# Sparse attention and two feed-forward layers on one core: an unrolled program with another order of slots

## The chip, the cores and the metric

The kernel runs on one core of a Trainium2 chip. Its time is the device time of that core in microseconds (us). The kernel before took 1284.62 us, the median of three runs (1283.78 to 1285.82). Every instruction duration below comes from one profiled execution of it.

## The reference

Four batches of eight heads with 576 tokens each and head dimension 64. Each row of scores keeps its 32 largest values; the rest get weight zero.

```
scores = (q @ k.T) / 8
kth    = partition(scores, -32)[..., -32]          # the 32nd largest of each row
scores = where(scores >= kth, scores, -1e9)
attn   = exp(scores - max) / (sum(exp(scores - max)) + 1e-9)
x  = (attn @ v) laid out as 2304 tokens x 512
h  = x @ w_in ;  g = h - tanh(h) ;  y = g @ w_out       # first feed-forward, 512 -> 2048 -> 512
h2 = y @ w_in2 ; g2 = elu(h2)    ;  out = g2 @ w_out2   # second feed-forward
```

Everything is in float32. The large products are made of three float32r products each (high by high, low by high, high by low), so every tensor that enters one is split into a high and a low part.

## The kernel before

The program has two phases. In the first, attention and the first feed-forward layer run side by side, in slots written out by hand; in the second, the second feed-forward layer runs alone (`h2`, `y2`, line 683 and line 728) over four groups of 512 tokens and one of 256.

A **unit** of attention is one tile of 128 queries of one head, against 576 keys; there are 144, one to a slot. The 64 queries that are left over in each head are gathered into tail units. Nine slots make a round, and each engine walks through its own list of every slot:

- TensorE (`round_`): turn the weights of unit u-3 with five transposes (`turn_weights`, lines 579 and 580), scores of unit u+1 (lines 563 and 564), some pieces of the first layer (`h_part` line 611, `y_part` line 626, transposes of g, line 653, and of x, line 647), and last weights by values of unit u-3 (`attend`, line 598).
- VectorE: four MAX8 and three MATCH_REPLACE8 find the 32 largest scores (lines 964, 973, 979, 984, 993, 1005). A reciprocal of the weight sum, which comes out of the product with an added column of ones, is line 989. It also makes h - tanh(h) for two of four blocks (line 998).
- ScalarE: exp of unit u-2 (line 821), copies out of PSUM (scores line 782, the rest through `high`, line 755), tanh (line 833), scaling of the attention's result by the reciprocal (line 865).
- GpSimd: the mask, scores >= 32nd (line 1104), exp times mask (line 1110), and low parts (lines 1076, 1092, 1122, 1131).

An engine runs its list strictly in its order; semaphores hold it where it needs another's result. The exp and the mask of a unit are made one slot before TensorE turns its weights. Steady slots are in loops (`Fori`); a tile of 128 tokens goes through the first layer in nine slots, with 512-wide products.

Of the kernel before, what the change touches and what calls it, by code (L numbers as in the profile page):

```python
# [6 lines left out]
F32R = mybir.dt.float32r  # L28
ALU = mybir.AluOpType
# [4 lines left out]
LOWEST = -3.0e38  # L34
EPS = 1e-9
# [5 lines left out]
def after(eng, sem, count):  # L41

    if not (isinstance(count, int) and count <= 0):
        eng.wait_ge(sem, count)


def apart(eng, passed):


    eng.sem_inc(passed)  # L50


class Round:

    def __init__(self, rho, batch, pair, rounds, units=True, refill=False, fresh=False, left=True, new=True, old=True):
        self.rho, self.batch, self.pair, self.refill, self.fresh = rho, batch, pair, refill, fresh
        self.pair_before = (pair + 3) % 4
        self.units, self.left, self.new, self.old = units, left, new, old
        self.more = units and not (isinstance(rho, int) and rho == rounds - 1)

    def has(self, u):

        if u < 0:
            return self.left
        return self.units if u < 9 else self.more


def each_round(eng, step, batches, tails):

    per = 4
    n = batches * per
    step(Round(0, 0, 0, n, left=False, new=False, old=False))  # L80
    step(Round(1, 0, 1, n, old=False))
    step(Round(2, 0, 2, n))
    step(Round(3, 0, 3, n, refill=True))
    with eng.Fori(1, batches - 1) as b:
        step(Round(b * per, b, 0, n, fresh=True))
        with eng.Fori(1, per - 1) as r:
            step(Round(b * per + r, b, r, n))
        step(Round(b * per + per - 1, b, per - 1, n, refill=True))
    step(Round(n - per, batches - 1, 0, n, fresh=True))
    with eng.Fori(1, per - 1) as r:  # L90
        step(Round(r + (n - per), batches - 1, r, n))
    step(Round(n - 1, batches - 1, per - 1, n))
    step(Round(n, batches, 0, n, units=False))
    for i in range(tails):
        step(Round(n + 1 + i, batches, 0, n, units=False, left=False))
    step(Round(n + 1 + tails, batches, 0, n, units=False, left=False, new=False))


def build(nc, qT, kT, v, w1_in, w1_out, w2_in, w2_out, out):
# [21 lines left out]
    with ctx:  # L121
# [131 lines left out]

        W2_SLOTS = {1: (0, 1, 2, 3)}
        OUT_AHEAD = 2

# [929 lines left out]
```

## Time and profile before

| | |
|---|---|
| median of 3 runs | 1284.62 us |
| span of the profiled execution | 1281.9 us |
| TensorE busy | 1203.8 us (94%) |
| VectorE busy | 896.5 us (70%) |
| ScalarE busy | 702.2 us (55%) |
| GpSimd busy | 790.3 us (62%) |
| first product of the second layer starts | 872.38 us |

The span leaves out about 3 us around the first and the last instruction. The busy share of TensorE is an upper figure: its matmuls overlap, and their modelled durations are longer than the distance from one start to the next. So distances between starts are what prices a product. Until about 780 us VectorE is full as well; after 872 us only TensorE is.

### The profile page before, as it was taken

Reading aid. Unit: us, or ns where it says so; the run is one execution under the profiler, and the core shown is the slowest. Engines: PE = TensorE matmul, PEld = TensorE weight load, DVE = VectorE, ACT = ScalarE, POOL = GpSimd, SP = SyncE. Lnnn points to the kernel's source line nnn. Section 1 sums busy time; section 2 is a strip of 40 time slices with the busy share of each in tenths; the row PEclk is TensorE's granted clock in tenths of the full one; section 3 lists DMA queues with packets and bytes.
Section 4 is the critical chain, followed back from the end, with each engine's and each line's share of the span. In section 5 each row is a group of like instructions: output and inputs, shape, how many; then the busy total and the mean of one; then the engine's idle time right before and its main releaser. Section 6 shows DMA issues by size and latency. Waiting matters only on the chain.

```text
span 1281.9 us, 23141 instructions
## 1 busy us (share of the span) xinstructions
PE 1203.8 (94%) x6784; PEld 1039.2 (81%) x6784; DVE 896.5 (70%) x1870; ACT 702.2 (55%) x1534; POOL 790.3 (62%) x579
## 2 busy tenths in 40 slices
PE   3678999999998999999999999999999999999997
PEld 2667887888887888888888888788888888888887
DVE  7999999999999999999999995015532222222221
ACT  5667777766776766777766765345432222222221
POOL 4898888888987888988888986332222222222221
PEclk9679999999999999999999999999999999999999
DMA  6410022000022100022000000504001001010000
GB/s 201 168 56 13 20 62 75 30 21 22 23 68 64 32 21 21 25 66 68 28 26 13 21 11 12 188 12 170 1 1 66 1 1 65 0 50 1 1 33 17
DMA packets 46420, 56.81 MB, mean 44 GB/s; under 512 B 13296, under 2 KB 28656, under 8 KB 45808
## 3 DMA queue, kind: packets, MB, share of 16 engines
q1 hardware_dynamic: 46320, 55.59, 13.7%
q8 instruction: 48, 0.79, 0.2%
q14 instruction: 52, 0.43, 0.1%
HBM read 45.61 MB, written 9.96 MB: 43 GB/s over the span
## 4 chain that ended last, share of the span: by engine, by line
PE 71%; issue 12%; DVE 6%; ACT 5%; POOL 4%; DVEq 0%; DMA 0%; ACTq 0%; POOLq 0%; SPq 0%
PE ps L683 15%; PE ps L728 15%; PE ps L611 11%; PE ps L626 10%; PE ps L598 9%; PE ps L579 4%; PE ps L563 2%; PE ps L564 2%; PE ps L653 2%; DVE best L973 1%; POOL keep L1104 1%; DVE work L1005 1%; DVE best L964 1%; PE ps L580 1%; ACT kT_hi_over_lo L755 1%
## 5 line engine op out<-in xcount | busy, mean ns | idle before, releaser
L1104 POOL TENSOR_SCALAR keep<-scores,best 128x576 f32<-128x576 f32 x144 | 253.6, 1761 | 58.3 <-DVE best L964 55.9
L1148 POOL TENSOR_TENSOR elu_lo<-elu_h,elu_hi 128x512 fp32r<-128x512 f32 x72 | 92.9, 1290 | 305.7 <-ACT elu_hi L755 305.7
L598 PEld LDWEIGHTS ps<-v_and_one,weights_T 128*128 128x128 f32 (+1 forms) x1440 | 183.5, 198 | 56.0 <-issue 49.3
L598 PE MATMUL ps<-v_and_one,weights_T 128*128 128x129 f32 (+2 forms) x1440 | 196.1, 285 | 34.9 <-ACT x L865 33.0
L1110 POOL TENSOR_TENSOR kept_weights<-work,keep 128x576 f32<-128x576 f32 x144 | 205.9, 1430 | 26.8 <-POOL keep L1104 17.8
L964 DVE MAX8 best<-work 128x8 f32<-128x576 f32 x288 | 213.8, 742 | 0.2
L1043 DVE TENSOR_SCALAR exp_h<-exp_h 128x512 f32<-128x512 f32 x72 | 30.7, 427 | 239.9 <-ACT exp_h L907 239.9
L755 ACT ACTIVATE weights_T<-ps 128x512 f32<-128x512 f32 (+1 forms) x288 | 115.1, 433 | 118.6 <-PE ps L580 105.1
L907 ACT ACTIVATE exp_h<-ps 128x512 f32<-128x512 f32 x72 | 43.1, 598 | 194.3 <-PE ps L683 194.3
L821 ACT ACTIVATE work<-scores,exp_bias 128x576 f32<-128x576 f32 x144 | 111.6, 775 | 24.4 <-DVE best L964 24.0
L563 PE MATMUL ps<-kT_hi_over_lo,qT_hi 128*128 128x288 f32 (+1 forms) x320 | 106.1, 347 | 20.1 <-DVE kT_hi_over_lo L937 15.5
L1122 POOL TENSOR_TENSOR gT_lo<-gT_raw,gT_hi 128x512 fp32r<-128x512 f32 x72 | 92.5, 1285 | 45.9 <-ACT gT_hi L755 45.1
L626 PE MATMUL ps<-w_out_hi,gT_hi 128*128 128x512 f32 x288 | 115.7, 402 | 2.8 <-POOL gT_lo L1122 2.5
L683 PE MATMUL ps<-yT_hi,w_in_hi 128*128 (+2 forms) x320 | 117.8, 368 | 0.0
L683 PE MATMUL ps<-yT_lo,w_in_hi 128*128 (+2 forms) x320 | 117.8, 368 | 0.0
L683 PE MATMUL ps<-yT_hi,w_in_lo 128*128 (+2 forms) x320 | 117.7, 368 | 0.0
L611 PE MATMUL ps<-w_in_hi,xT_hi 128*128 128x512 f32 x288 | 115.4, 401 | 0.0
L728 PE MATMUL ps<-w_out_hi,elu_hi 128*128 128x512 f32 x288 | 113.6, 395 | 1.1 <-POOL elu_lo L1148 1.1
L973 DVE MAX8 best<-scores 128x8 f32<-128x576 f32 x144 | 108.4, 753 | 8.0 <-ACT scores L782 4.7
L611 PE MATMUL ps<-w_in_hi,xT_lo 128*128 128x512 f32 x288 | 112.9, 392 | 0.0
L611 PE MATMUL ps<-w_in_lo,xT_hi 128*128 128x512 f32 x288 | 112.8, 392 | 0.0
L626 PE MATMUL ps<-w_out_lo,gT_hi 128*128 128x512 f32 x288 | 112.5, 391 | 0.0
(83 smaller groups left out, 2880.7 us busy)
## 6 DMA issues: line engine op xcount, KB each, us to landing
kT_raw<-kT SPq DMA_DIRECT2D x64, 144.0 KB, 2.8
w_in_raw<-w_in SPq DMA_DIRECT2D x8, 1024.0 KB, 7.5
w_out_raw<-w_out SPq DMA_DIRECT2D x8, 1024.0 KB, 5.5
qT_raw<-qT SPq DMA_DIRECT2D x64, 96.0 KB, 2.5
ffn_rows<-act SPq DMA_DIRECT2D x18, 256.0 KB, 2.1
v_and_one<-v SPq DMA_DIRECT2D x16, 256.0 KB, 2.7
rows<-ffn_rows SPq DMA_DIRECT2D x4, 1024.0 KB, 6.5
out<-out_rows SPq DMA_DIRECT2D x16, 256.0 KB, 2.4
```

The costliest lines, as they stand in the source:

```text
L563: pe.matmul(ps[:, half, 0:HALF], q_hi[:, slot, :], rhs, start=(n == 0), stop=False)
L598: mm = pe.matmul(ps[:, B_OUT, 0:2 * D + 1], pt[0:k, c, :], rhs, start=(c == 0), stop=(c == FULL))
L611: mm = pe.matmul(ps[:, B_H + fb % 2, :], l[:, kc, :], r[:, kc, ws], start=(kc == 0 and n == 0), stop=(kc == KC - 1 and n == 2))
L626: mm = pe.matmul(ps[:, B_Y, :], l[:, fb % 2, c, :], r[:, fb * CPB + c, :], start=(fb == 0 and c == 0 and n == 0), stop=(fb == FB - 1 and c ...
L683: mm = pe.matmul(ps[:, B_H + f % 2, j * n * P:(j + 1) * n * P], l[:, kc, cs], r(kc), start=(kc == 0 and i == 0), stop=(kc == KC - 1 and i ...
L728: mm = pe.matmul(ps[:, t, :], l[:, f % 2, ts], r[:, c, :], start=(c == 0 and i == 0), stop=(c == FC - 1 and i == 2))
L755: return nc.scalar.activation(out_, in_, ACT.Copy)
L821: nc.scalar.activation(wk[:, i, :], sc[:, i, :], ACT.Exp, bias=nbias[:, i:i + 1], scale=SCALE).then_inc(exped, 1)
L964: nc.vector.max(best[:, u % 3, n * EIGHT:(n + 1) * EIGHT], wk[:, u % 3, :]).then_inc(chain_old, 1)
L973: nc.vector.max(best[:, i, 0:EIGHT], sc[:, i, :]).then_inc(chain_new, 1)
L1104: nc.gpsimd.tensor_scalar(keep[:, :], sc[:, i, :], best[:, i, TOP - 1:TOP], None, ALU.is_ge).then_inc(kept, 1)
L1110: nc.gpsimd.tensor_tensor(kept_w[:, :], wk[:, i, :], keep[:, :], ALU.mult).then_inc(masked, 1)
```

## The change

The whole program is written anew, without loops. There are again 144 attention slots (128 head tiles, 16 tail units, four of these after the first tile of each batch), numbered from 0.

- **Mask.** The comparison and the product with the mask are gone. GpSimd makes two small differences per unit (`biases`: minus the 32nd score, and the 32nd score minus the maximum); ScalarE runs a Prelu over the scores with the first as bias and a slope of 1e30 below zero (`cut_scores`), then exp in place, which also gives the sum of the weights (`exp_scores`, `accum_out`). GpSimd adds 1e-9 (`sum_eps`), VectorE inverts (`invert`), GpSimd multiplies the weights by the inverse (`norm`).
- **Order of a slot on TensorE:** scores of the next unit, attend of a finished pair, one chunk of h, one chunk of y, and last the turn of the weights.
- **Values.** attend runs for a pair of heads at once, with 64 columns of values as the stationary operand and the turned weights streaming, into upper and lower halves of one bank. Its result is x already transposed, so the transposes of x are gone.
- **First layer.** h comes out transposed, for two tiles at a time (256 columns streaming); the transposes of g are gone. One chunk of h and one of y per slot, in slots 24 to 168: 144 chunks.
- **Elsewhere.** The low parts of the first weights are all made by GpSimd, two in each of slots 5 to 20; the low parts of the keys of later batches by GpSimd too (24). The copy of scores applies the scale. The second layer's own steps stay the same; half of its weights' splits are placed elsewhere.

The core of the difference, TensorE's list of a slot and the new steps:

```diff
-                for u in range(U):
-                    if rd.has(u - 3):
-                        turn_weights(rd, u - 3)
-                    if rd.has(u + 1) and rd.units:
-                        scores(rd, u + 1)
-                    for step, fb, first, end, which in steps(rd, u):
...
-                    if rd.has(u - 3):
-                        attend(rd, u - 3)
+            for s in range(-1, LAST + 1):
+                done, old, new = unit(s - 3), unit(s - 2), unit(s + 1)
+                if new:
+                    scores(new)
+                if done and done.ends_pair:
+                    attend(done)
+                if s in h_in:
+                    h_step(h_in[s])
+                if s in y_in:
+                    y_step(y_in[s])
+                if old:
+                    turn_weights(old)
```

```diff
-                        nc.gpsimd.tensor_scalar(keep[:, :], sc[:, i, :], best[:, i, TOP - 1:TOP], None, ALU.is_ge
-                                                ).then_inc(kept, 1)
...
-                        nc.gpsimd.tensor_tensor(kept_w[:, :], wk[:, i, :], keep[:, :], ALU.mult).then_inc(masked, 1)
+            def cut_scores(u):
+                sc_e.wait_ge(biased, u.t + 1)
+                nc.scalar.activation(sc[:, u.t % 4, :], sc[:, u.t % 4, :], ACT.Prelu, bias=bias[:, u.t % 2, 0:1],
+                                     scale=1.0, alpha=STEEP).then_inc(cut, 1)
+            def exp_scores(u):
+                sc_e.wait_ge(cut, u.t + 1)
+                after(sc_e, summed, u.t - 1)
+                nc.scalar.activation(sc[:, u.t % 4, :], sc[:, u.t % 4, :], ACT.Exp, bias=bias[:, u.t % 2, 1:2],
+                                     scale=1.0, accum_out=sums[:, u.t % 2:u.t % 2 + 1]).then_inc(exped, 1)
+            def norm(u):
+                po.wait_ge(inverted, u.t + 1)
+                w = sc[:, u.t % 4, :]
+                nc.gpsimd.tensor_scalar(w, w, rinv[:, u.t % 2:u.t % 2 + 1], 1.0, ALU.mult, ALU.mult).then_inc(normed, 1)
+            def turn_weights(u):
+                pe.wait_ge(normed, u.t + 1)
```

```diff
+            def attend(u):
...
+                        mm = pe.matmul(ps[half * D:(half + 1) * D, B_OUT, cols], values[:, half * D:(half + 1) * D],
+                                       weights, start=(c == 0), stop=(c == FULL))
+            def h_step(i):
...
+                for kc in range(KC):
+                    for n, (l, r) in enumerate(((win_hi, xt_hi), (win_lo, xt_hi), (win_hi, xt_lo))):
+                        mm = pe.matmul(ps[:, B_H + i % 2, 0:N], l[:, kc, fs], r[:, kc, ring:ring + N],
+                                       start=(kc == 0 and n == 0), stop=(kc == KC - 1 and n == 2))
```

ScalarE's list, one steady slot of the kernel before (loops' register rows are among them). `work` is the exp, `weights_T` the turned weights of the unit before it, `gT` the first layer's g:

```order
L815 ACTIVATE exp_bias<-best 128x1 [waits chain_new]
L819 ISA
L821 ACTIVATE work<-scores,exp_bias 128x576 [waits biased,chain_old]
L755 ACTIVATE weights_T<-ps 128x512 [waits attended,turned]
L839 REGISTER_ALU
L755 ACTIVATE weights_T<-ps 64x128 [waits scored]
L755 ACTIVATE gT_raw<-ps 128x512 [waits y_done,g_turned]
L755 ACTIVATE gT_hi<-ps 128x512
L865 ACTIVATE x<-ps,sum_inverse 128x64 [waits inverted]
```

And of the changed kernel, from the cut of a unit (L607) to the cut of the next:

```order
L607 ACTIVATE scores<-scores,exp_bias 128x576 [waits biased]
L580 ACTIVATE gT_hi<-gT_raw 128x256 [waits g_done]
L613 ACTIVATE scores,weight_sum<-scores,exp_bias 128x576 [waits summed,cut]
L602 ACTIVATE scores<-ps 128x576 [waits turned,scored]
L580 ACTIVATE gT_raw<-ps 128x256 [waits y_done,h_done]
L647 ACTIVATE tanh_h<-ps 128x256
L580 ACTIVATE weights_T<-ps 128x512 [waits attended,turned]
L580 ACTIVATE weights_T<-ps 64x128
L607 ACTIVATE scores<-scores,exp_bias 128x576 [waits biased]
```

The copy of turned weights stood behind the exp of a younger unit; now it is the last step of the slot in which the same unit was cut and exponentiated, and the next unit's cut stands behind it.

GpSimd's list in the same place, one slot of the kernel before (the mask of a unit, then its weights):

```order
L1104 TENSOR_SCALAR keep<-scores,best 128x576 [waits chain_old,masked]
L1107 REGISTER_ALU
L1110 TENSOR_TENSOR kept_weights<-work,keep 128x576 [waits kept,turned,exped]
L1119 REGISTER_ALU
L1122 TENSOR_TENSOR gT_lo<-gT_raw,gT_hi 128x512 [waits split_high]
```

And of the changed kernel, a slot in which queries are split too:

```order
L907 TENSOR_TENSOR gT_lo<-gT_raw,gT_hi 128x256 [waits g_high]
L893 TENSOR_SCALAR weight_sum_eps<-weight_sum 128x1 [waits inverted,exped]
L861 TENSOR_TENSOR qT_lo<-qT_raw,qT_hi 128x256 [waits q_high]
L898 TENSOR_SCALAR scores<-scores,sum_inverse 128x576 [waits inverted]
L902 TENSOR_TENSOR gT_raw<-gT_raw,tanh_h 128x256 [waits tanh_done]
L886 TENSOR_TENSOR exp_bias<-best 128x2 [waits exped,chain_late]
```

Where one full-width pass took the threshold from VectorE and the other the exp from ScalarE, the one full-width pass (L898) now waits for VectorE's reciprocal, which waits for L893.

TensorE in a slot that ends a pair, changed kernel (`v_rows` and `v_rest` are the values):

```order
L436 MATMUL ps<-kT_hi_over_lo,qT_hi 128x288 [waits copied,k_split,q_split]
L437 MATMUL ps<-kT_hi_over_lo,qT_lo 128x288
L436 MATMUL ps<-kT_hi_over_lo,qT_hi 128x288
L437 MATMUL ps<-kT_hi_over_lo,qT_lo 128x288
L464 MATMUL ps<-weights_T,v_rows 64x128 [waits x_out,turned_copied,v_in2]
L464 MATMUL ps<-weights_T,v_rows 64x128 x7
L464 MATMUL ps<-weights_T,v_rest 64x128 x2
L483 MATMUL ps<-xT_hi,w_in_hi 128x256 [waits turned_copied,tanh_done]
```

The turn of the weights has moved from the head of the slot to its end, and attend, ten products every second slot in place of five in each, from the end to behind the scores.

## Rows read from the trace of the kernel before

**Rows 1.** The page: span, and busy time by engine.

```profile
span 1281.9 us, 23141 instructions
PE 1203.8 (94%) x6784; PEld 1039.2 (81%) x6784; DVE 896.5 (70%) x1870; ACT 702.2 (55%) x1534; POOL 790.3 (62%) x579
```

**Rows 2.** Stretches: width, busy us and instructions by engine, TensorE's granted clock, DMA, GB/s.

```profile
40.00:80.00 40.00, 28.11 (x134) 25.25 (x134) 39.34 (x82) 26.35 (x61) 37.70 (x27) 0.63 0.37 131
...
480.00:520.00 40.00, 39.36 (x258) 35.21 (x257) 40.00 (x91) 28.20 (x68) 35.73 (x26) 1.00 0.06 18
```

**Rows 3.** The chain that ended last, in order of time: start, us, what.

```profile
486.32 0.44 PE ps L579 x4
...
487.40 2.74 PE ps L611 x12
490.14 0.44 PE ps L653 x4
490.57 1.12 PE ps L598 x10
```

**Rows 4.** The same chain, where the second layer begins.

```profile
872.38 2.77 PE ps L683 x12
```

**Rows 5.** VectorE in order of time: start, busy us, operation; first unit, then one steady unit.

```profile
10.27 0.76 DVE L973 MAX8 best<-scores 128x8 f32<-128x576 f32 x1 [0.30 <-ACT scores L782]
...
500.48 0.75 DVE L973 MAX8 best<-scores 128x8 f32<-128x576 f32 x1
...
505.37 0.74 DVE L973 MAX8 best<-scores 128x8 f32<-128x576 f32 x1
```

**Rows 6.** ScalarE by line and shape: count, busy us, mean ns.

```profile
L821 ACT ACTIVATE work<-scores,exp_bias 128x576 f32<-128x576 f32 x144 | 111.6, 775 | 24.4 <-DVE best L964 24.0
L755 ACT ACTIVATE weights_T<-ps 128x512 f32<-128x512 f32 x144 | 85.9, 597 | 106.2 <-PE ps L580 105.1
L833 ACT ACTIVATE act<-ps 128x512 f32<-128x512 f32 x72 | 42.7, 592 | 4.5 <-PE ps L611 4.4
L755 ACT ACTIVATE weights_T<-ps 64x128 f32<-64x128 f32 x144 | 38.7, 269 | 12.4 <-PE ps L564 12.4
L755 ACT ACTIVATE qT_hi<-qT_raw 128x256 fp32r<-128x256 f32 x16 | 6.7, 419 | 0.0
```

**Rows 7.** GpSimd and VectorE by line and shape.

```profile
L1104 POOL TENSOR_SCALAR keep<-scores,best 128x576 f32<-128x576 f32 x144 | 253.6, 1761 | 58.3 <-DVE best L964 55.9 <-POOL kept_weights L1110 1.4 <-POOL kT_hi_over_lo L1092 0.9
L1076 POOL TENSOR_TENSOR qT_lo<-qT_raw,qT_hi 128x256 fp32r<-128x256 f32 x16 | 12.2, 763 | 0.0
L1133 POOL MEMSET qT_hi<- 128x256 f32 x1 | 0.3, 311 | 0.3 <-POOLq L1183 0.3
L989 DVE RECIPROCAL sum_inverse<-ps 128x1 f32<-128x1 f32 x144 | 22.5, 156 | 10.3 <-PE ps L598 10.3
```

**Rows 8.** GpSimd, two low parts of weights.

```profile
37.38 2.84 POOL L1131 TENSOR_TENSOR w_in_lo<-w_in_raw,w_in_hi 128x512 fp32r<-128x512 f32 x2 [3.36 <-ACT w_in_hi L755]
```

**Rows 9.** Hand-overs from engine to engine, in order of time.

```profile
499.10 0.74 DVE L964 MAX8 best<-work 128x8 f32<-128x576 f32 x1
...
500.07 1.72 POOL L1104 TENSOR_SCALAR keep<-scores,best 128x576 f32<-128x576 f32 x1 [0.79 <-DVE best L964]
...
501.46 0.27 PE L580 MATMUL ps<-ident,kept_weights 128*64 128x128 f32 x1
501.85 0.75 ACT L755 ACTIVATE weights_T<-ps 128x512 f32<-128x512 f32 x2 [1.20 <-PE ps L580]
...
1226.59 0.63 ACT L755 ACTIVATE elu_hi<-elu_h 128x512 fp32r<-128x512 f32 x1 [1.22 <-DVE elu_h L1048]
1227.30 1.29 POOL L1148 TENSOR_TENSOR elu_lo<-elu_h,elu_hi 128x512 fp32r<-128x512 f32 x1 [4.15 <-ACT elu_hi L755]
```

**Rows 10.** TensorE, 256-column products of the last group; the 1st and the 13th.

```profile
1227.30 0.28 PE L683 MATMUL ps<-yT_hi,w_in_hi 128*128 128x256 f32 x1
...
1228.73 0.28 PE L683 MATMUL ps<-yT_hi,w_in_hi 128*128 128x256 f32 x1
```

More of the change, by code:

```diff
@@ L34 @@
 LOWEST = -3.0e38
+STEEP = 1.0e30
 EPS = 1e-9
@@ L41, in after, with __init__, plan @@
 def after(eng, sem, count):
-    if not (isinstance(count, int) and count <= 0):
+    if count > 0:
         eng.wait_ge(sem, count)
[L47 to L96, printed above, removed]
+class Unit:
+    def __init__(self, t, batch, tile, head=None, pair=None):
+        self.t, self.batch, self.tile, self.head, self.pair = t, batch, tile, head, pair
+        self.tail = head is None
+        self.ends_pair = self.tail or head % 2 == 1
+def plan(batches, per, heads):
+    units = []
+    for b in range(batches):
+        for r in range(per):
+            for h in range(heads):
+                units.append(Unit(len(units), b, b * per + r, head=h, pair=h // 2))
+            if r == 0:
+                for p in range(heads // 2):
+                    units.append(Unit(len(units), b, None, pair=p))
+    return units
 def build(nc, qT, kT, v, w1_in, w1_out, w2_in, w2_out, out):
@@ new lines, in build @@
+    last_unit_of = {u.tile: u.t for u in units if not u.tail}
+    for u in units:
+        if u.tail:
+            last_unit_of[R + u.batch // 2] = u.t
+    tiles = sorted(range(TILES), key=last_unit_of.get)
+    seq_of = {tile: j for j, tile in enumerate(tiles)}
+    RING = 4
+    GN = 2
+    GROUPS = TILES // GN
+    N = GN * P
+    CHUNKS = GROUPS * FC
+    READY = 5
+    h_slot = []
+    for g in range(GROUPS):
+        first = max(last_unit_of[tiles[g * GN + GN - 1]] + READY, h_slot[-1] + 1 if h_slot else 0)
+        h_slot += range(first, first + FC)
@@ L720, in y2 @@
                     after(pe, res_dve, g * (CPB // 2))
-                if isinstance(g, int) and g == 0:
+                if g == 0:
                     pe.wait_ge(w2o_split, f + 1)
@@ new lines, in copy_x @@
+            def copy_x(u):
+                e = event_of[u.t]
+                sc_e.wait_ge(attended, e + 1)
+                if u.tail:
+                    half = u.batch % 2
+                    if u.pair == 0 and half == 0 and u.batch > 0:
+                        sc_e.wait_ge(x_split, seq_of[R + u.batch // 2 - 1] + 1)
+                    to = tail_raw[:, u.pair, half * D:(half + 1) * D]
+                    high(to, ps[:, B_OUT, 0:D]).then_inc(x_out, 1)
+                else:
+                    if u.pair == 0 and u.tile > 0:
+                        sc_e.wait_ge(x_split, seq_of[u.tile - 1] + 1)
+                    high(tile_raw[:, u.pair, :], ps[:, B_OUT, 0:P]).then_inc(x_out, 1)
```

1151 lines of the change are left out of this document (501 added, 650 removed).

## The prediction

> **What bounds the kernel now.** I read the page's busy times first, then the table of stretches, then the chain of waits in order of time, and last the engines' own timelines for the distance between starts. TensorE is busy for 94% of the span and VectorE for 70% [rows 1]. In a stretch in the middle of the first phase both are full: VectorE 40.00 of 40.00 us, TensorE 39.36, at the full clock [rows 2]. The chain there is nothing but TensorE: from a turn to the end of the next attend 5.37 us (486.32 to 491.69), made of 1.08 for the turn and the scores (486.32 to 487.40), 2.74 for twelve 512-column products, 0.44 for turning g and 1.12 for ten passes of attend [rows 3]. One unit costs VectorE 4.89 us (500.48 to 505.37) where no block of g falls to it [rows 5]. So a slot is worth 5.0 to 5.4 us, held by TensorE with VectorE close behind; ScalarE and GpSimd have room, and no unit's exp, mask and turn fall into one slot. The first unit starts at 10.27 [rows 5], the second layer at 872.38 [rows 4]; its remaining 409.5 us stay as they are.
>
> **TensorE's and VectorE's work in the changed kernel.** Thirteen starts of 256-column products lie 1.43 us apart over twelve [rows 10], so a chunk of h costs 1.43. A chunk of y is six products at 2.74/12 = 0.228, 1.37. With turn and scores 1.08 and attend at the old price, 1.12 a unit, a slot holds 5.0 us of TensorE: as much as before, since the saved transposes (0.44, two or three times in nine slots) are paid for by 256-column products, which cost 0.119 for half of what costs 0.228. VectorE keeps seven passes and a reciprocal, 4.89, and loses the blocks of g. If these two set the pace, the kernel gains. I don't think they do.
>
> **The wait that the order adds.** In the changed kernel ScalarE's list of a slot begins with the cut of a unit and ends with the copy of that same unit's turned weights, and the next unit's cut stands behind that copy. Between them lies everything: cut, exp, sum, reciprocal, norm, turn, copy. That is a closed loop of one slot, and its length is a sum of rows:
> cut 0.68 (0.775, Prelu priced as exp, less the 0.10 by which neighbours overlap in the pair of copies of [rows 9]: 0.75 for 0.597 + 0.269); high part of g 0.32 (0.419 less 0.10); exp 0.775 [rows 6]; its sum 0.15, which no row shows: I take half of the smallest copy, 0.269, with 0 and 0.27 as ends; hand-over to GpSimd 0.08 (1226.59 + 0.63 to 1227.30 [rows 9]); the addition on 128 x 1 an estimated 0.20 (the 128x256 row, 0.763, is the nearest above); hand-over 0.08; reciprocal 0.156 [rows 7]; VectorE to GpSimd 0.23 (499.84 to 500.07 [rows 9]); norm n; hand-over 0.08; turn 0.71 (0.44 for four [rows 3] and the fifth's 0.27); to ScalarE 0.12 (501.73 to 501.85); copies 0.67. Sum: 4.25 + n.
> For n, a one-tensor pass of 576 elements on GpSimd, the rows give 1.761 for the comparison, also one tensor and a pointer, as the upper end, and for the lower a memset scaled from 256 to 576 elements, 0.70 [rows 7]. A product needs no comparison; I take 1.3. The loop is then 5.55 us, over both engines' work.
> That functions cost the same on ScalarE is in [rows 6]: tanh on 512 elements 592 ns, copy 597. So Prelu's price is hardly in doubt.
> The page GPSIMD Engine Reference of the Trainium skill (section Engine selection) says that one-input passes on GpSimd are "roughly line-rate". The trace disagrees for the comparison: 1.761 for 576 elements is 3.1 ns an element [rows 7], and a two-input subtraction of 512, 1.29 us, is 2.5 [rows 9]. With a line-rate norm of about 0.6 us, an estimate from that page, the time below would be near 1365.
>
> **Two kinds of slots.** Odd slots: the low part of the queries, 0.763, stands in GpSimd's list between the sum and the norm, where only 0.47 (0.08 + 0.156 + 0.23) is free, so they cost 0.30 more, 5.85. Even slots end a pair: TensorE, after its turn, waits for the copy (0.12 + 0.77 + 0.08), then attend, h, y and turn follow in a row: 0.97 + 1.43 + 1.37 + 0.71 = 4.48 plus attend. Twenty passes at 1.12/10 make 2.24, if halves of the array don't work at once, 1.12 if they do. No row shows two column halves side by side. I take 1.6, between the ends: 6.08. The mean is 5.96 us a slot.
> TensorEngine Tiling (Array Packing) in the Trainium skill (section Key Properties) says that different tiles of the array run independently; by that rule attend costs 1.12 and the sum is that of the first rival below. No row here shows it either way.
>
> **The sum.** Slots 0 to 4 and 21 to 23, without g: 5.23 each, 42. Slots 5 to 20: GpSimd makes two low parts of weights, 2.84 [rows 8], between norm and the next biases, so its own loop is 2.84 + 0.25 (biases, estimate) + 0.08 + cut 0.83 + exp 0.93 + 0.08 + 0.20 + 0.08 + 0.16 + 0.23 + 1.3 = 6.98, times 16 = 112. With the start at 10.3, slot 24 begins at 164. Slots 24 to 145: 122 x 5.96 = 727. To these come the low parts of 24 keys, priced as one of a weight, 1.42 each [rows 8], and again between sum and norm: 15 fall on odd slots in full, 9 on even ones for about 0.4, 25 us; and 16 low parts of x at 1.29 (the 512-wide row of [rows 9]), all on odd slots, 21. Attention ends at 937. Then 22 slots hold h and y alone: work 2.80, and the way h, tanh, difference, high part, low part, y about 3.0, which with two buffers makes 2.9 a slot, 64; last y 1.4; then 409.5. Together 1412 on the profiled execution's clock; the median lies 2.7 over the span [rows 1], so 1415 us.
> Edits priced at nothing: the longer list of ScalarE, 3 us of it inside its wait for the turn, which is 3.4 long; splits of the second weights, two passes on ScalarE and two on VectorE a slot in the last 12 slots, where VectorE has nothing else to do; queries' and values' loads on SP, waited for two slots or more after issue; the loops' register work, saved, on engines that have time. If ScalarE's cover is gone, in slots with keys (1.2 more), the cost is some tenths on 24 slots, under 10 us.
>
> **Rivals.**
> *Halves side by side and a cheap norm* (0.17): even slots 5.60, odd ones 5.25 at n = 0.7, and about the same fixed parts less 12: near 1340 with no price for the sum, 1389 where n stays 1.3. For it: nothing in the trace forbids either. Against it: each needs the lower end.
> *The loop doesn't bind, VectorE does* (0.08, the side on which the kernel is faster): if ScalarE's and GpSimd's steps overlap more than their rows do, a slot costs VectorE's 4.89 and 146 of them end at 10 + 714 + 20 for the slots with weights = 744; with 64 + 1.4 + 409.5 + 2.7 that is 1222 us. The place is ScalarE's copy of turned weights, and it decides from a mean of 5.27 us over slots 24 to 145, extras included: (1284.6 - 2.7 - 409.5 - 65.4 - 164)/122. Against it: 4.25 + n gives 4.95 even at n = 0.70, and queries, keys and x come on top of that in the same place.
> *No overlap and a dear norm* (0.15): attend 2.24, n = 1.761: even 6.72, odd 6.31, 122 x 6.52 = 795, start 11 more: 1490 us.
> *The clock falls* (0.04): TensorE would be idle for 15 to 20% of each slot. In 40 to 80 us, with 28.11 of 40 busy, the granted clock was 0.63 of full speed [rows 2], which is the 1.2 GHz level for much of it. At that level the slot's 5.0 us become 10: every ten slots add 40 us, so over 1500. Against it, such stretches would have to last.
>
> **How the numbers follow.** Forecast 0.56: the loop binds, with prices between the ends. It gives 1415. Range 1340 to 1490, from the low ends of norm and attend to their high ends, which leaves out the fast rival and the clock. What a measurement can tell from no change is 0.2%, about 2.6 us. Slower: 0.91, that is forecast, first, third and fourth rival, less 0.01 for a mean slot that lands just on 5.27. Faster 0.08, same 0.01.
>
> **What would show it.** Right: in the profile after, VectorE idles before each reciprocal, about 0.7 to 1.1 us, waiting for GpSimd; ScalarE idles before the copy of turned weights, released by TensorE's turn; TensorE idles before the turn in odd slots, released by GpSimd's norm; starts of MAX8 on scores lie 5.8 to 6.1 apart. The chain walks cut, exp, norm, turn, copy. Slots 5 to 20 are near 7 us. The norm's mean and the distance of attend's passes decide the size. Wrong: VectorE full between 170 and 900 us, or a chain that is all TensorE.

## The result and the profile after

| | before | changed |
|---|---|---|
| median, us | 1284.2 (1282.85 to 1285.82, 4 runs) | 1471.07 (1469.05 to 1472.4, 4 runs) |
| ratio to before | | 1.1458, 95% interval 1.1442 to 1.1474 |
| profiled execution: span, us | 1281.9 | 1467.2 |
| mean granted clock of TensorE | 0.980 | 0.934 |

The kernel became 14.6% slower. The forecast was 1415 us, its range 1340 to 1490.

The page of the changed kernel: busy time by engine, then three groups of the page (busy us, mean ns | idle before, releaser).

```profile
PE 1214.2 (83%) x7448; PEld 1001.5 (68%) x7448; DVE 846.8 (58%) x1796; ACT 767.9 (52%) x1792; POOL 624.1 (43%) x968
...
L580 ACT ACTIVATE weights_T<-ps 128x512 f32<-128x512 f32 (+1 forms) x288 | 108.2, 427 | 220.1 <-PE ps L448 220.1
...
L447 PE MATMUL ps<-ident,scores 128*128 128x128 f32 x576 | 101.5, 304 | 121.5 <-POOL scores L898 121.0
...
L792 DVE RECIPROCAL sum_inverse<-weight_sum_eps 128x1 f32<-128x1 f32 x144 | 23.5, 163 | 202.9 <-POOL weight_sum_eps L893 202.9
...
L898 POOL TENSOR_SCALAR scores<-scores,sum_inverse 128x576 f32<-128x576 f32 x144 | 108.4, 753 | 25.1 <-DVE sum_inverse L792 23.9
```

Against [rows 1]: TensorE's work is nearly the same (1214.2 us for 1203.8), VectorE's, ScalarE's and GpSimd's together is 150 us less, and the span is 185 us longer: 177 of it ahead of the second layer, whose first product starts at 1049.40 and not 872.38 [rows 4], and 8 in it. In the attention slots no engine is full any more. The three waits that the prediction named are all there: ScalarE before the copy of turned weights (220.1 us), TensorE before the turn (121.5), VectorE before the reciprocal (202.9).

The stretches that answer to [rows 2], one in the slots with weights' splits and one in the middle:

```profile
120.00:160.00 40.00, 20.48 (x135) 16.65 (x134) 32.05 (x72) 28.27 (x62) 25.30 (x38) 0.59 0.04 11
...
480.00:520.00 40.00, 31.12 (x216) 25.39 (x216) 28.34 (x62) 29.61 (x71) 21.62 (x36) 0.91 0.18 52
```

VectorE, 40.00 of 40 before in the second of them, is at 28.34.

One odd slot in the changed kernel, from ScalarE's cut to the next. These are lines of the trace in order of time, each engine's own (start, busy us, operation, idle before it and who ended it). ScalarE:

```profile
437.48 0.75 ACT L580 ACTIVATE weights_T<-ps 128x512 f32<-128x512 f32 x2 [1.28 <-PE ps L448]
438.13 0.77 ACT L607 ACTIVATE scores<-scores,exp_bias 128x576 f32<-128x576 f32 x1
438.80 0.41 ACT L580 ACTIVATE gT_hi<-gT_raw 128x256 fp32r<-128x256 f32 x1
439.11 0.77 ACT L613 ACTIVATE scores<-scores,exp_bias 128x576 f32<-128x576 f32 x1
439.77 0.20 ACT L613 ACTIVATION_READ_ACCUMULATOR scores<-scores,exp_bias 128x1 f32 x1
...
442.73 0.75 ACT L580 ACTIVATE weights_T<-ps 128x512 f32<-128x512 f32 x2 [1.69 <-PE ps L448]
443.38 0.77 ACT L607 ACTIVATE scores<-scores,exp_bias 128x576 f32<-128x576 f32 x1
```

GpSimd, with the low part of the queries (L861) between sum and norm:

```profile
440.11 0.21 POOL L893 TENSOR_SCALAR weight_sum_eps<-weight_sum 128x1 f32<-128x1 f32 x1
440.40 0.74 POOL L861 TENSOR_TENSOR qT_lo<-qT_raw,qT_hi 128x256 fp32r<-128x256 f32 x1
441.12 0.75 POOL L898 TENSOR_SCALAR scores<-scores,sum_inverse 128x576 f32<-128x576 f32 x1
```

TensorE, the even slot before and this odd one's turn:

```profile
432.42 1.09 PE L464 MATMUL ps<-weights_T,v_rows 128*64 128x128 f32 x16 [0.36 <-issue]
433.44 0.44 PE L464 MATMUL ps<-weights_T,v_rest 64*64 64x128 f32 x4
433.81 0.39 PE L483 MATMUL ps<-xT_hi,w_in_hi 128*128 128x256 f32 x1
...
435.35 0.40 PE L497 MATMUL ps<-w_out_hi,gT_hi 128*128 128x512 f32 x1
...
436.74 0.60 PE L447 MATMUL ps<-ident,scores 128*128 128x128 f32 x4
...
441.93 0.66 PE L447 MATMUL ps<-ident,scores 128*128 128x128 f32 x4 [0.19 <-POOL scores L898]
```

Odd slot: copy done 438.13, cut, high part, exp from 439.11, accumulator read to 439.97, sum at 440.11, queries' low part, norm at 441.12, turn at 441.93, copy at 442.73, next cut at 443.38: 5.25 us, all of it one strand through ScalarE, GpSimd and TensorE. Even slot: copy 431.57 (not shown), attend 432.42, h 433.81, y 435.35, turn 436.74, copy 437.48: 5.91, and from the copy on it is TensorE's own work. Between the cuts of slots 24 and 145 lie 121 distances. 77 of them are plain: mostly 5.2 and 5.9 us in turn, 4.8 to 6.1 in all. The other 44, all above 6.2, are treated below. One unit took 4.89 before [rows 5].

### The profile page after: what moved, and what is told of

Read it like the earlier page. It is cut to its first block, busy times and chain, and to the rows that moved or that the text cites. A ratio compares the mean times of both kernels' runs of the same rounds, so it can differ in the third digit from the quotient of the medians.

```text
span 1467.2 us, 21851 instructions
## 1 busy us (share of the span) xinstructions
PE 1214.2 (83%) x7448; PEld 1001.5 (68%) x7448; DVE 846.8 (58%) x1796; ACT 767.9 (52%) x1792; POOL 624.1 (43%) x968
## 4 chain that ended last, share of the span: by engine, by line
PE 34%; POOL 29%; issue 26%; ACT 3%; DVE 3%; SPq 2%; DMA 1%; POOLq 0%; ACTq 0%
PE ps L544 13%; PE ps L527 13%; POOL gT_lo L907 6%; POOL scores L898 6%; POOL gT_raw L902 5%; POOL qT_lo L861 3%; PE ps L497 2%; POOL kT_hi_over_lo L868 2%; PE ps L483 2%; POOL weight_sum_eps L893 2%; PE ps L464 2%; POOL exp_bias L886 1%; POOL xT_lo L880 1%; DVE best L776 1%; DVE work L785 1%
## 5 line engine op out<-in xcount | busy, mean ns | idle before, releaser
L580 ACT ACTIVATE weights_T<-ps 128x512 f32<-128x512 f32 (+1 forms) x288 | 108.2, 427 | 220.1 <-PE ps L448 220.1
L785 DVE MATCH_REPLACE8 work<-best,work 128x576 f32<-128x576 f32 x288 | 213.9, 743 | 0.0
L447 PE MATMUL ps<-ident,scores 128*128 128x128 f32 x576 | 101.5, 304 | 121.5 <-POOL scores L898 121.0
L483 PE MATMUL ps<-xT_hi,w_in_hi 128*128 128x256 f32 x576 | 177.2, 308 | 22.4 <-ACT weights_T L580 22.4
L483 PE MATMUL ps<-xT_hi,w_in_lo 128*128 128x256 f32 x576 | 165.3, 287 | 0.0
L483 PE MATMUL ps<-xT_lo,w_in_hi 128*128 128x256 f32 x576 | 164.9, 286 | 0.0
L436 PE MATMUL ps<-kT_hi_over_lo,qT_hi 128*128 128x288 f32 x320 | 115.2, 373 | 42.1 <-POOL qT_lo L861 27.5
L483 PEld LDWEIGHTS ps<-xT_hi,w_in_hi 128*128 128x128 f32 x576 | 112.1, 195 | 45.0 <-issue 37.3
L792 DVE RECIPROCAL sum_inverse<-weight_sum_eps 128x1 f32<-128x1 f32 x144 | 23.5, 163 | 202.9 <-POOL weight_sum_eps L893 202.9
L607 ACT ACTIVATE scores<-scores,exp_bias 128x576 f32<-128x576 f32 x144 | 110.8, 770 | 27.5 <-POOL exp_bias L886 27.5
L527 PE MATMUL ps<-yT_hi,w_in_hi 128*128 128x512 f32 (+1 forms) x320 | 119.8, 374 | 0.0
L527 PE MATMUL ps<-yT_lo,w_in_hi 128*128 128x512 f32 (+1 forms) x320 | 119.3, 373 | 0.0
L898 POOL TENSOR_SCALAR scores<-scores,sum_inverse 128x576 f32<-128x576 f32 x144 | 108.4, 753 | 25.1 <-DVE sum_inverse L792 23.9
L527 PE MATMUL ps<-yT_hi,w_in_lo 128*128 128x512 f32 (+1 forms) x320 | 119.1, 372 | 0.0
```

The costliest lines, as they stand in the source:

```text
L436: pe.matmul(ps[:, half, 0:HALF], q_hi[:, n % QRING, lhs], rhs, start=(i == 0), stop=False)
L447: pe.transpose(ps[:, B_TURN, c * P:(c + 1) * P], w[:, c * P:(c + 1) * P], ident[:, :])
L483: mm = pe.matmul(ps[:, B_H + i % 2, 0:N], l[:, kc, fs], r[:, kc, ring:ring + N], start=(kc == 0 and n == 0), stop=(kc == KC - 1 and n == 2))
L527: mm = pe.matmul(ps[:, B_H + f % 2, j * n * P:(j + 1) * n * P], l[:, kc, cs], r[:, buf, kc, 0:n * P], start=(kc == 0 and i == 0), stop=(kc ...
L607: nc.scalar.activation(sc[:, u.t % 4, :], sc[:, u.t % 4, :], ACT.Prelu, bias=bias[:, u.t % 2, 0:1], scale=1.0, alpha=STEEP).then_inc(cut, 1)
L785: nc.vector.match_replace(wk[:, u.t % 2, :], best[:, u.t % 3, 1 + n * EIGHT:1 + (n + 1) * EIGHT], src, LOWEST).then_inc(chain if n < 2 els ...
```

## The experiments

Each was timed beside the kernel before in three rounds. The last columns are read off each profiled execution: the start of the cut of unit 22 (slot 24), the time from it to the cut of unit 143 (slot 145), and the distances of cuts in plain odd and even slots.

| kernel | median | ratio to before | unit 22 | 22 to 143 | odd / even |
|---|---|---|---|---|---|
| changed kernel | 1471.07 | 1.1458 [1.1442, 1.1474] | 186.2 | 777.8 | 5.2 / 5.9 |
| norm_twice | 1533.51 | 1.1945 [1.1923, 1.1968] | 198.5 | 830.7 | 6.0 / 5.9 |
| halves_apart | 1559.28 | 1.2154 [1.2121, 1.2187] | 199.1 | 855.4 | 5.2 / 7.2 |
| cut_first | 1514.82 | 1.1811 [1.1786, 1.1837] | 200.4 | 809.2 | 5.3 / 6.3 |
| turn_before_y | 1472.77 | 1.1477 [1.1454, 1.1499] | 186.0 | 781.5 | 5.2 / 6.0 |
| y_early | 1453.81 | 1.1328 [1.1309, 1.1347] | 187.1 | 767.3 | 5.2 / 5.9 |
| w_late | 1452.80 | 1.1325 [1.1306, 1.1344] | 170.4 | 777.8 | 5.2 / 5.9 |
| norm_first | 1451.31 | 1.1306 [1.1287, 1.1325] | 188.6 | 760.4 | 4.8 / 5.9 |
| all_six | 1506.60 | 1.1735 [1.1715, 1.1755] | 187.3 | 816.2 | 5.5 / 6.3 |
| biases_first | 1466.66 | 1.1426 [1.1407, 1.1445] | 188.1 | 774.2 | 5.2 / 5.9 |
| cut_and_biases_first | 1443.35 | 1.1263 [1.1229, 1.1297] | 200.3 | 733.1 | 5.4 / 5.2 |
| turn_and_biases_first | 1436.02 | 1.1186 [1.1168, 1.1205] | 187.3 | 746.0 | 5.2 / 5.5 |
| three_out | 1417.48 | 1.1038 [1.1020, 1.1056] | 171.5 | 744.8 | 4.8 / 5.9 |

**norm_twice: is it a loop through GpSimd?** A second product by 1.0 stands behind the norm, and the turn waits for both.

```diff
+                po.wait_ge(normed, 2 * u.t + 1)
+                nc.gpsimd.tensor_scalar(w, w, 1.0, 1.0, ALU.mult, ALU.mult).then_inc(normed, 1)
```

> The multiplication of the weights by the inverse sum runs twice on GpSimd (the second time by 1.0), so 0.75 us and a hand-over of 0.18 more between reciprocal and turn, in every attention slot; nothing else changes. Theory A (odd slots are held by the one-slot loop cut, exp, sum, reciprocal, norm, turn, copy, cut; even slots, which end a pair, by TensorE's own chain, in which the norm is over 1.3 us before the turn): the 61 odd slots from 24 on grow from 5.2-5.3 to about 6.15 us, even ones stay at 5.9, the first 24 slots and those with keys grow by up to 0.9: 1471 becomes 1540 to 1560 us. Theory B (TensorE's work and its waits for turned weights hold all slots, GpSimd is covered): under 10 us more.

GpSimd in this kernel, an odd slot:

```profile
437.21 0.75 POOL L898 TENSOR_SCALAR scores<-scores,sum_inverse 128x576 f32<-128x576 f32 x1 [0.30 <-DVE sum_inverse L792]
438.04 0.67 POOL L900 TENSOR_SCALAR scores<-scores 128x576 f32<-128x576 f32 x1
```

The second pass starts 0.83 us behind the first. Plain odd slots grew by 0.8 (5.2 to 6.0), and even slots in the regular succession not at all. So the loop holds the odd slots, with no slack, and TensorE the even ones. GpSimd's whole busy share had been 43%: the added 0.8 us cost 62 us because of where they stand, 53 of them after unit 22. The time is 6.5 us under the expected range. Plain odd slots gave 25 of the 53 us; five even slots behind a low part of x gave 11 (5.9 to between 7.0 and 8.8), which I had not expected, and the seven group ends and three batch starts gave nothing.

**halves_apart: do the column halves work at once?** attend goes through one head's ten passes, then the other's, in place of the two in turn.

```diff
-                for c in range(FULL + 1):
-                    k = P if c < FULL else REST
-                    for half in (0, 1):
+                for half in (0, 1):
+                    for c in range(FULL + 1):
+                        k = P if c < FULL else REST
```

> The two loops in attend change places: all five chunks of the lower half of the array's columns, then all five of the upper, instead of taking turns. The same twenty passes. If the 1.39 us of attend come from two column halves at work at once, it goes back to about 20 x 0.11 = 2.2 us, and the 61 even slots, held by TensorE, grow by 0.8: about 1520 us. If attend is short because weights of 64 columns load faster, nothing changes: 1471.

```profile
653.13 1.06 PE L464 MATMUL ps<-weights_T,v_rows 128*64 128x128 f32 x8 [0.36 <-issue]
654.12 0.43 PE L464 MATMUL ps<-weights_T,v_rest 64*64 64x128 f32 x2
654.48 1.09 PE L464 MATMUL ps<-weights_T,v_rows 128*64 128x128 f32 x8
655.50 0.43 PE L464 MATMUL ps<-weights_T,v_rest 64*64 64x128 f32 x2
```

Eight passes take here as long (1.09) as sixteen in the changed kernel at 432.42. Twenty are 2.7 us instead of 1.39, and each even slot grew by that 1.3, which is more than the 0.8 that I had taken; hence 1559 us and not 1520. A pass behind one in the same half starts 0.11 us later, which is also the distance of full-width transposes (0.44 for four [rows 3]); so weights of 64 columns by themselves save nothing. In the changed kernel two passes start in each 0.11 us. The two halves do run together; only with the order by head they don't. This bears out the rule of TensorEngine Tiling (Array Packing) in the Trainium skill, section Key Properties, that tiles of the array work independently, for column halves: 1.39 us against 1.12 for ten passes of a unit before [rows 3].

**cut_first: take the cut out of the loop.** The next unit's cut before the copy of turned weights instead of behind it.

```diff
-                if old:
+                if s == 2:
                     cut_scores(old)
...
+                if s >= 2 and unit(s - 1):
+                    cut_scores(unit(s - 1))
                 if old:
                     copy_turned(old)
```

> ScalarE cuts the next unit before it copies this slot's turned weights, so the cut (0.68) falls into its wait for TensorE's turn. Theory A: the one-slot loop is 0.6 shorter, odd slots go from 5.25 to VectorE's floor of 4.9, even ones stay: 20 to 35 us less, 1436 to 1450. Theory B (TensorE's chain holds all slots): unchanged, within 5 us.

It lost 44 us where 20 to 35 should have been won. ScalarE in the trace:

```profile
621.39 0.78 ACT L607 ACTIVATE scores<-scores,exp_bias 128x576 f32<-128x576 f32 x1 [1.00 <-POOL exp_bias L888]
622.08 0.73 ACT L580 ACTIVATE weights_T<-ps 128x512 f32<-128x512 f32 x2
```

and GpSimd just before:

```profile
619.24 0.74 POOL L900 TENSOR_SCALAR scores<-scores,sum_inverse 128x576 f32<-128x576 f32 x1
...
620.47 0.73 POOL L904 TENSOR_TENSOR gT_raw<-gT_raw,tanh_h 128x256 f32<-128x256 f32 x1 [0.49 <-ACT tanh_h L647]
...
621.17 0.19 POOL L888 TENSOR_TENSOR exp_bias<-best 128x2 f32<-128x2 f32 x1
```

The cut doesn't only need its scores: its biases are GpSimd's last piece of the slot, behind norm and the difference of g, and the difference waits for h and its tanh. They ended at 621.36, the turn at 621.63. The cut so began just before the copy could have, and pushed it back from there to 622.08, by 0.4: that is what the even slots grew by. There are two strands from the norm to the next exp, one over turn and copy, one over difference, biases and cut, and they are nearly equally long. I had seen only the first.

**turn_before_y: the norm's result used sooner.** The turn stands ahead of the second product's chunk on TensorE.

```diff
-                if s in y_in:
-                    y_step(y_in[s])
                 if old:
                     turn_weights(old)
+                if s in y_in:
+                    y_step(y_in[s])
```

> TensorE turns the weights before the chunk of y, no longer last. Theory A: in even slots the turn can begin at the end of the norm, 1.2 us earlier, and the copy, which the next unit's cut waits for, with it; in odd slots TensorE waits about 2 us for the norm before y instead of behind it, but the next scores are not what anybody waits for. A pair of slots goes from 11.1 to about 10.2 us: 50 to 60 us less, about 1415. Theory B: TensorE's list is as long as before and its wait for the norm now stands before y as well: unchanged to 60 us slower.

Nothing moved (1.1477 against 1.1458, intervals overlapping), where 55 us were expected. ScalarE, an even slot:

```profile
449.05 0.38 ACT L580 ACTIVATE gT_raw<-ps 128x256 f32<-128x256 f32 x1 [1.04 <-PE ps L483]
449.33 0.38 ACT L647 ACTIVATE tanh_h<-ps 128x256 f32<-128x256 f32 x1
449.60 0.75 ACT L580 ACTIVATE weights_T<-ps 128x512 f32<-128x512 f32 x2
450.72 0.78 ACT L607 ACTIVATE scores<-scores,exp_bias 128x576 f32<-128x576 f32 x1 [0.37 <-POOL exp_bias L886]
```

The turn was done before the copy could begin, because ScalarE had h's evacuation and tanh first; and then the cut waited 0.37 us for the biases. Again the second strand.

That nothing moved is a sum of two effects. At the seven group ends, where the turn no longer stands behind a y that waits (see y_early below), each such slot and the one behind it became shorter, by 17 us in all; the other slots from 24 on became 21 us longer. About half of that lies in even slots behind a low part of x, for example 7.5 us for 5.9 in slot 52: in the slot before, TensorE waited 2.8 us for the norm, now with y behind it, and so came late to the next scores and attend.

```profile
376.03 0.28 ACT L580 ACTIVATE tile_xT<-ps 128x128 f32<-128x128 f32 x1 [1.28 <-PE ps L464]
```

The expectation had that wait in it and called it harmless.

**biases_first, alone and with each of these two.** On GpSimd the biases ahead of the difference, which they don't depend on.

```diff
-                if s in h_in:
-                    difference(h_in[s])
                 if old:
                     biases(old)
+                if s in h_in:
+                    difference(h_in[s])
```

> GpSimd forms a unit's biases ahead of the slot's difference instead of behind it (0.74 us earlier). Control. Theory (in the changed kernel the cut stands behind the copy of the turned weights, and the biases are done about a microsecond before that copy ends): no change, 1471 within 5 us, cuts still 5.2 and 5.9 us apart. Rival (the strand norm, difference, biases, cut already holds a part of the slots): 1471 less 0.2 to 0.7 in every second slot, 1430 to 1458.

> The cut ahead of the copy of the turned weights, and the biases ahead of the difference. Theory (the cut moved alone lost because the biases came only behind norm and difference, so that the cut began when the turn ended and pushed the copy back): now the biases end 0.2 us behind the norm, while TensorE turns or is still at the second product; the cut is mostly hidden and 0.5 to 0.6 us go from each of 122 slots: 1390 to 1415. Rival (what was lost came of the copy, and so attend, standing behind the cut, wherever the cut begins): 1505 to 1520, slots 5.3 and 6.3.

> The turn ahead of the second product's passes, and the biases ahead of the difference. Theory (the moved turn gained nothing since in even slots the cut then waited 0.37 us for biases that stood behind a later difference): 0.3 to 0.4 us go from every second slot, 1445 to 1460. Rival (the h passes, their tanh and the copy behind it set the even slot, biases or not): 1471 within 5 us.

Alone it left the plain slots at 5.2 and 5.9; its 4 us lie in other slots. With the cut moved, the same edit is worth 71 us (1514.82 to 1443.35), with the turn moved 37 us (1472.77 to 1436.02). Both rivals, in which the copy or h's passes alone decided, fall. cut_and_biases_first, GpSimd and then ScalarE at one odd and one even slot:

```profile
435.13 0.20 POOL L888 TENSOR_TENSOR exp_bias<-best 128x2 f32<-128x2 f32 x1
435.28 0.73 POOL L904 TENSOR_TENSOR gT_raw<-gT_raw,tanh_h 128x256 f32<-128x256 f32 x1
```

```profile
435.36 0.78 ACT L607 ACTIVATE scores<-scores,exp_bias 128x576 f32<-128x576 f32 x1 [0.73 <-POOL exp_bias L888]
436.04 0.73 ACT L580 ACTIVATE weights_T<-ps 128x512 f32<-128x512 f32 x2
...
440.53 0.78 ACT L607 ACTIVATE scores<-scores,exp_bias 128x576 f32<-128x576 f32 x1
...
441.92 0.75 ACT L580 ACTIVATE weights_T<-ps 128x512 f32<-128x512 f32 x2 [0.61 <-PE ps L448]
```

In even slots the cut is now hidden, with 0.61 us to spare before the copy (5.9 to 5.2). In odd ones it still waits for the biases behind queries and norm, so those don't gain (5.2 to 5.4). That is one miss: I had expected 0.5 to 0.6 of each slot. The other is the start. Unit 22 is cut 14 us later than in the changed kernel: in slots 5 to 20 the biases come behind 2.5 us of weights' low parts, and a copy behind that cut joins GpSimd's loop, which makes 6.9 us of 6.2 (cuts at 120.73 and 127.64). So 1443 instead of 1390 to 1415. turn_and_biases_first missed on the other side, 1436 for 1445 to 1460. Its plain even slots lost 0.5 against turn_before_y (6.0 to 5.5), a little more than expected, 19 us together; most of the rest came off slots of irregular kinds, which it hadn't counted.

**y_early: the group ends.** Both tiles of a group leave their y through one buffer (`y_rows`). That stays so; the first tile's y is now copied at the head of ScalarE's slot.

```diff
+                if y_in.get(s - 1, 0) % FC == FC - 1:
+                    copy_y(y_in[s - 1] // FC, 0)
                 if old:
...
-                if y_in.get(s - 1, 0) % FC == FC - 1:
-                    copy_y(y_in[s - 1] // FC, 0)
```

> At the end of a group of two tiles, ScalarE copies the first tile's y out at the very beginning of the slot, not behind exp and the copy of scores; the second copy needs the same buffer and waits until the first is saved. Theory: the slots of 10 to 12 us that come once in a group (eight of them) are this wait: the save takes about 2 us, TensorE's next y waits for both copies, and the turn stands behind that y. With the first copy 2.5 us earlier, each of these slots loses 2 to 3 us: 16 to 25 us less, about 1450. Rival (the long slots come from the low parts of x or of keys on GpSimd): no change.

As expected, within 4 us. What it shortens is in the changed kernel's trace at a group's end:

```profile
609.17 0.58 ACT L580 ACTIVATE y_rows<-ps 128x512 f32<-128x512 f32 x1
...
609.78 3.07 SPq L349 DMA_DIRECT2D ffn_rows<-y_rows  x2
...
611.89 0.60 ACT L580 ACTIVATE y_rows<-ps 128x512 f32<-128x512 f32 x1 [1.59 <-DMA ffn_rows<-y_rows]
...
612.63 0.77 PE L497 MATMUL ps<-w_out_hi,gT_hi 128*128 128x512 f32 x1 [3.81 <-ACT y_rows L580]
...
614.90 0.63 PE L497 MATMUL ps<-w_out_hi,gT_lo 128*128 128x512 f32 x1
615.33 1.05 PE L447 MATMUL ps<-ident,scores 128*128 128x128 f32 x4
...
616.63 0.75 ACT L580 ACTIVATE weights_T<-ps 128x512 f32<-128x512 f32 x2 [4.15 <-PE ps L448]
```

The second copy waits 1.59 us for the first one's transfer, the next y waits 3.81 for that copy, the turn stands behind y, and the slot is 10.4 us long. TensorE's own passes are also slower behind that idle time: y's starts lie 0.43 us apart instead of 0.23, and four transposes take 1.05 instead of 0.60. The granted clock was 0.50 there, the 1.2 GHz level, and 1.00 again from 618 to 620:

```profile
614.00:616.00 2.00, 2.00 (x8) 1.56 (x7) 0.10 (x1) 0.00 (x0) 0.00 (x0) 0.50 0.03 9
```

From the start of y to the start of the copy it is 4.00 us here (612.63 to 616.63) against 2.13 in the even slot above (435.35 to 437.48), so by estimate about 1.9 us of this slot's excess is the clock. Of the seven such slots between units 22 and 143 six got 1.3 to 3.9 us shorter in y_early; slot 105 did not.

**w_late: the start.** SP issues one piece of the first weights per slot instead of all before slot -1.

```diff
-            for i in range(2 * FB):
-                load_weights(i)
+            load_weights(0)
             for s in range(-1, LAST + 1):
+                if 1 <= s <= 2 * FB - 1:
+                    load_weights(s)
```

> Seven of the eight loads of the first weights (1 MB each) are issued one to a slot from slot 1 on, behind that slot's predecessors in the list, and no longer all before the fourth group of queries. Theory: the stall of 25 us between the first and the second cut is the queries waiting behind 8 MB; it goes, and 15 to 22 us of it stay gone, since the weights are needed from slot 5 on and now come later: about 1450. Rival (the loads as such fill the queues until about 45 us whatever their order, and the weights' splits in slots 5 to 20 wait instead): under 5 us less.

As expected, within 3 us: unit 22 is 16 us earlier, the distance from there the same. In the changed kernel ScalarE's first long wait was

```profile
45.99 0.42 ACT L580 ACTIVATE qT_hi<-qT_raw 128x256 fp32r<-128x256 f32 x1 [18.39 <-DMA qT_raw<-qT]
```

and in w_late it is

```profile
29.70 0.42 ACT L581 ACTIVATE qT_hi<-qT_raw 128x256 fp32r<-128x256 f32 x1 [2.02 <-DMA qT_raw<-qT]
```

The load of these queries was issued from 33.56 on in the changed kernel, behind eight transfers of 1 MB each in SP's list, and its last part landed at 45.97, as the last of those had at 45.62.

**norm_first: the odd slots.** The norm directly behind the sum, ahead of the low parts.

```diff
                     sum_eps(exped_u)
+                    norm(exped_u)
...
-                if exped_u:
-                    norm(exped_u)
```

> GpSimd multiplies the weights right behind the sum, before the low parts of keys, x and queries. Theory A: in odd slots 0.5 us less in the loop, which VectorE's 4.89 cuts to about 0.35; the slots with keys and x lose up to 1.4 to 2.7 us each: together 40 to 60 us less, about 1420. Theory B (TensorE's chain holds all slots): under 10 us less.

Odd slots became 4.8, 0.4 less, as expected; the next limit was reached, VectorE's unit: here two starts of MAX8 with an odd slot between them, 4.88 apart as in [rows 5].

```profile
667.08 0.75 DVE L776 MAX8 best<-scores 128x8 f32<-128x576 f32 x1
...
671.96 0.75 DVE L776 MAX8 best<-scores 128x8 f32<-128x576 f32 x1
```

But it is 20 us in all for about 51 expected. The missing part is in the slots with keys, which were to lose up to 1.4 to 2.7 us. Seven even ones grew by 1.1 to 2.1 (slot 36: 6.8 to 7.9), since the low part of the keys now stands behind the norm and ScalarE waits for it with the next keys, ahead of h and the copy of turned weights; this wait was 1.02 us in the changed kernel:

```profile
266.41 0.68 ACT L580 ACTIVATE kT_hi_upper<-kT_raw 64x576 fp32r<-64x576 f32 x1 [2.05 <-POOL kT_hi_over_lo L868]
```

**all_six and three_out: do gains add?** all_six holds the five edits cut_first, turn_before_y, norm_first, y_early and w_late together.

> Five edits together: the cut before the copy, the turn before y, the first copy of y early, the weights' loads late, the norm first. If the one-slot loop, the group's end and the start explain the loss, slots come near VectorE's 4.9 to 5.1: 122 x 5.1 = 622 for slots 24 to 145, with 160 ahead, 75 behind and 418 for the second layer about 1275 to 1310 us. If TensorE's chain holds, no better than 1380.

It is far off, 1506.6. Its plain slots are 5.5 and 6.3, no better than cut_first's 5.3 and 6.3, and ScalarE waits 229 us for the biases (213 in cut_first): with the second strand in charge, edits to the first one gain nothing in these slots. three_out leaves out the two edits that gained nothing.

> Three edits that gained by themselves in one kernel: copies of y at the head of ScalarE's slot with a buffer each (-17), the 8 MB weights' loads one a slot (-18), the norm ahead of GpSimd's low parts (-20). Theory (they are three separate delays: at the group ends, at the start, in the odd slots): their gains add, 1471 - 55 = 1416, 1408 to 1424. Rival (the last edit's gain is partly at the group ends too, or TensorE's slots take over): 1430 to 1445.

1417.48: the sum of three single gains, 17 + 18 + 20, was 1416. (The y copies share one buffer here too, as in y_early.) This is the best of the changed program's versions that ran, and still 10.4% above the kernel before. A version with the biases moved as well, in all of these, was not run.

## Why the prediction was right, and where it was off

The side, the place and the mechanism held; the time is 56 us above the forecast and inside the range. By stretches, the 56 us are 22 at the start, 11 from slot 24 to the end of attention, 14 in the slots with h and y alone, 8 in the second layer, and 1 that comes of comparing different executions. That the long middle stretch is off by only 11 is luck, as the steps show:

- **The loop binds: right for odd slots.** Shown by norm_twice: +0.8 us on GpSimd, +0.8 a slot. Its predicted fixed parts, 4.25 + 0.30 for the queries, are 4.5 in the trace (5.25 less the norm's 0.75). The accumulator's read, taken as 0.15, is an instruction of 0.20 of its own that overlaps exp by 0.1.
- **Norm n = 1.3: too dear.** It is 0.753 us, near the lower end. That alone makes odd slots 5.3 for 5.85, and MAX8 starts lie 5.2 and 5.9 us apart, not 5.8 to 6.1. The estimate of 0.6 from the Trainium skill (GPSIMD Engine Reference, section Engine selection, one-input passes "roughly line-rate") was closer than my value: the trace has 1.3 ns an element for this product, and 3.1 for the comparison of [rows 7], so the rule agrees with the one and not with the other.
- **Even slots are TensorE's chain: right.** 5.91 for 6.08. attend 1.39 for 1.6 (halves_apart shows why), h to y 1.54 for 1.43.
- **Mean plain slot** so 5.6, not 5.96 (77 of the 121 slots from unit 22 to 143 take 430.1 us): the first rival's mechanism, halves together and a cheap norm, is what happened, and its plain slots (5.60 and 5.25) are within 0.3 us of the measured ones. That its time of 1340 is missed by 131 us is due to all that follows. The forecast's own premise, both prices between the ends, did not hold for the norm, which sits at the low end.
- **"To these come ...": the term that failed.** I priced keys and x at 46 us and nothing else. The other 44 slots of those 121 take 347.7 us; at 5.59 each they would take 246, so the extras are about 102. Keys and x were priced about right: 37 in 23 slots, 14 in eleven slots that follow special ones. What was left out are two kinds, 51 us: seven group ends of 9 to 10.6 us (31; y_early took 10.5 off the 777.8), and three slots of about 12 at the start of a batch (20). There TensorE's scores waited 4.9 us for the queries' low part (its line of the trace below), which stands in GpSimd's list behind the low part of x while the scores that need it are due at once. No experiment took that one away. Keys with x and queries in one slot cost 8.0 to 8.6, since three low parts (1.43, 1.26 and 0.73) stand between sum and norm.

```profile
340.38 0.61 PE L436 MATMUL ps<-kT_hi_over_lo,qT_hi 128*128 128x288 f32 x1 [4.94 <-POOL qT_lo L861]
```

- **Start: slot 24 begins at 164: off by 22.** Most slots with weights are 6.2, not 6.98 (two low parts 2.5 instead of 2.84, the cheap norm), but slots 10 and 11 take 9.2 and 10.7, since TensorE's scores wait up to 7.9 us for a low part of queries; all sixteen take 107 us for 112. Slots 0 to 4 end 26 us later than priced. I had called the loads on SP "waited for two slots or more after issue" and priced them at nothing. The 18.4 us wait for queries is that sentence's error: I took the distance in slots, and not what stands ahead in SP's list. w_late shows it.
- **Slots with h and y alone:** last y at 1049 where 1003 would follow from 937; from the last attention slot on 79 us for 65. TensorE waits 2.2 us for the copy of y there and 1.8 for the last low part of g; the rest I did not trace.
- **"Its remaining 409.5 us stay as they are":** 417.8. The second layer's first own steps had stood between blocks of the first layer, and now nothing fills that hole: TensorE waits 1.9 us there, and its products start 0.43 us apart at first. Later on they start 0.23 to 0.24 apart where before it was mostly 0.227; why, I did not trace.
- **The clock rival** did not come true as a whole, though its cause exists: the granted clock was 0.59, near the 1.2 GHz level, in 120 to 160 us, where TensorE was busy for half of the time and waited up to 5.2 us for the norm, and 0.91 in 480 to 520, with 31.12 of 40 us busy. At the group end shown under y_early it was 0.50, and an estimate from the rows there gives it about 1.9 us of that slot. No run takes the clock's share away by itself.
- **VectorE decides (the fast side):** norm_first reached it in odd slots alone, 4.88. For the whole kernel a mean of 5.27 was needed; cut_and_biases_first's plain slots (5.3) come near, and the extras would still have to go.
- **Sums.** By their own terms the first rival at n = 1.3 gives 1386 us, not 1389, the third 1494, not 1490, and the line-rate norm 1356, not 1365. The profiled execution's time lies 1.85 us above its own span (1469.05 and 1467.2); the 2.7 that was added, and the 3 us of the section on time before, compare a median with the span of another execution.

So two errors of opposite sign met in the sum: plain slots 0.4 us too long, special slots at less than half of what they cost.

## What to carry to other kernels

When one engine's list of a step begins and ends with the same item's first and last link, the length of that whole way over all engines is the least time of a step, whatever the engines' busy shares are (here 5.25 us, with no engine over 80% busy in the middle of the phase); compare it with the busiest engine before choosing the order. Before moving one link out of such a loop, list the second-longest way to the same instruction, above all small ones that stand last in another engine's list: here the place of a 0.2 us subtraction decided over 71 us. And price every slot of an irregular kind by laying its lists side by side, in-order DMA queues included, since 44 special slots cost as much above the plain ones as 18 plain slots.

## What the runs showed of the hardware

- Column halves of TensorE (64 columns each) run at once when their passes alternate: sixteen passes of 128 columns in 1.09 us, as long as eight passes of one half (halves_apart).
- A tensor_scalar with two products on GpSimd takes 0.753 us for 576 elements, and one with immediate numbers 0.67; the comparison with a pointer of the kernel before took 1.761 [rows 7]. Both read one tensor, and the one comparison beside which VectorE was idle for most of the time took 1.72 all the same, so neither the number of inputs nor VectorE made the 2.3 times; what is left is the operation, or that the product is written in place, which no run separates.
- TensorE's 512-column products start 0.43 us apart at a granted clock of 0.50 (614 to 616) and 0.23 at 1.00.
- ScalarE's `accum_out` is an instruction of its own in the trace (ACTIVATION_READ_ACCUMULATOR, 0.19 to 0.20 us), beginning 0.1 us before the exp ends.
- Prelu with a pointer bias costs what exp costs: 770 and 768 ns for 576 elements.
